# A three-stage token kernel: first tile's side channels spread by ScalarE, late weights loaded over two turns, the last tile's second layer moved to the first layer's buffers

## What is computed

```python
x_unf = x_pad[:, idx, :].reshape(B, S, K, H, group)   # seven shifted copies
x = np.einsum('hk,bskhg->bshg', softmax(weight), x_unf).reshape(B * S, 192)
h = x @ w_in                  # layer one: 192 -> 2048
x = (h * np.cos(h)) @ w_out   # 2048 -> 192
h = np.maximum(x @ w_in2, 0)  # layer two: 192 -> 2048
out = (h * h) @ w_out2        # 2048 -> 192
```

## Time and profile before

| | us |
|---|---|
| runs of the kernel, median of 3 | 2283.05 (2282.98 to 2283.62) |
| the profiled execution: its own time | 2284.51 |
| the profiled execution: its span, first to last instruction | 2282.7 |
| busy in the span: PE, DVE, ACT | 2237.8 (98%), 1779.4 (78%), 1695.5 (74%) |
| mean granted clock of TensorE | 0.994 of full speed |

### The profile page before, as it was taken

How to read it: one execution, slowest core, us unless ns; L and a number is a source line. 1 busy time by engine, 2 the same in 40 slices (tenths; PEclk the granted TensorE clock), 3 DMA queues, 4 the chain that set the end, 5 groups by cost and what they waited for, 6 DMA issues and landing times.

```text
span 2282.7 us, 47134 instructions
## 1 busy us (share of the span) xinstructions
PE 2237.8 (98%) x19456; PEld 1855.2 (81%) x19456; DVE 1779.4 (78%) x2003; ACT 1695.5 (74%) x1747; POOL 0.2 (0%) x4
## 2 busy tenths in 40 slices
PE   5899999999999999999999999999999999999998
PEld 4688888888888888888888888888888888888887
DVE  7877887777887778887778877778877778877762
ACT  5577777777777777777777777777777777777775
POOL 0000000000000000000000000000000000000000
PEclk9899999999999999999999999999999999999999
DMA  3100000000000000000000000000000000000000
GB/s 103 58 12 20 20 7 18 18 12 18 18 7 18 18 12 18 18 7 18 16 14 18 12 13 18 12 18 18 8 17 18 12 18 18 7 18 18 5 8 15
DMA packets 23696, 41.57 MB, mean 18 GB/s; under 512 B 3952, under 2 KB 12144, under 8 KB 23408
## 3 DMA queue, kind: packets, MB, share of 16 engines
q1 hardware_dynamic: 23520, 41.11, 6.5%
q10 hardware_dynamic: 144, 0.01, 0.0%
HBM read 20.13 MB, written 12.58 MB: 14 GB/s over the span
## 4 chain that ended last, share of the span: by engine, by line
PE 95%; DVE 2%; ACT 1%; DMA 1%; issue 0%; SPq 0%; DVEq 0%
PE h L316 10%; PE h L322 10%; PE h L320 10%; PE h L318 10%; PE y_B L353 5%; PE y_B L357 5%; PE y_B L359 5%; PE y_B L355 5%; PE y_B L361 5%; PE h L325 5%; PE y_A L353 5%; PE y_A L361 5%; PE y_A L359 5%; PE y_A L355 5%; PE y_A L357 5%
## 5 line engine op out<-in xcount | busy, mean ns | idle before, releaser
L586 DVE TENSOR_TENSOR g_lo<-g,g_hi 128x1024 fp32r<-128x1024 f32 x512 | 625.4, 1222 | 271.5 <-ACT g_hi L466 270.0
L466 ACT ACTIVATE g_hi<-g 128x1024 fp32r<-128x1024 f32 x512 | 537.3, 1050 | 41.6 <-DVE g L582 41.6
L458 ACT ACTIVATE w<-w,quarter 128x1024 f32<-128x1024 f32 x256 | 295.0, 1152 | 272.7 <-DVE w L576 272.7
L353 PE MATMUL y_A<-g_hi,dn_lo_A 64*128 64x512 f32 x1024 | 399.7, 390 | 9.8 <-DVE g_lo L586 9.8
L359 PE MATMUL y_A<-g_hi,dn_side_A 64*128 64x512 f32 x1024 | 398.5, 389 | 0.0
L355 PE MATMUL y_A<-g_hi,dn_hi_A 64*128 64x512 f32 x1024 | 398.1, 389 | 0.0
L361 PE MATMUL y_A<-g_lo,dn_side_A 64*128 64x512 f32 x1024 | 398.1, 389 | 0.0
L353 PE MATMUL y_B<-g_hi,dn_lo_B 64*128 64x512 f32 x1024 | 397.4, 388 | 0.4
L357 PE MATMUL y_A<-g_lo,dn_hi_A 64*128 64x512 f32 x1024 | 397.8, 388 | 0.0
L359 PE MATMUL y_B<-g_hi,dn_side_B 64*128 64x512 f32 x1024 | 396.9, 388 | 0.0
L355 PE MATMUL y_B<-g_hi,dn_hi_B 64*128 64x512 f32 x1024 | 396.4, 387 | 0.0
(11 more groups left out here) (85 smaller groups left out, 6082.7 us busy)
## 6 DMA issues: line engine op xcount, KB each, us to landing
xt<-x SPq DMA_DIRECT2D x32, 390.0 KB, 3.2
conv_both<-conv_side SPq DMA_DIRECT2D x128, 64.0 KB, 2.1
out<-late SPq DMA_DIRECT2D x32, 256.0 KB, 2.0
out<-late SPq DMA_DIRECT2D x32, 128.0 KB, 2.3
late<-w_out SPq DMA_DIRECT2D x2, 1536.0 KB, 10.2
late<-w_in SPq DMA_DIRECT2D x2, 512.0 KB, 4.2
late<-w_in SPq DMA_DIRECT2D x4, 256.0 KB, 5.6
w<-w_in SPq DMA_DIRECT2D x1, 768.0 KB, 6.7
```

What stands on the lines that cost most here:

```text
L353: mm = pe.matmul(y[kind][:, 0, :], dn_lo[kind][rows, c, :], hi, start=a, stop=False)
L466: act.activation(g_hi[:, s % RING, :, :], g[:, s % RING, :, :], ACT.Copy).then_inc(hi_made[kind], 1)
L586: dve.tensor_tensor(g_lo[:, r, :, :], g[:, r, :, :], g_hi[:, r, :, :].bitcast(F32), ALU.subtract).then_inc(lo_made[kind], 1)
```

## The change

Three edits. (1) In turn -1 the side channels of tile 0 are no longer unfolded by four DMAs but by six ScalarE copies of 64 partitions by 256 columns (`first_split`), which write `conv_both` and the rounded `x_side_A` directly; ScalarE's work on layer one's weights is put in another order around it, and the sine's table is loaded by a dummy instruction before it. VectorE's low parts of layer one's down weights move from turn -1 to behind the fractions of the first two A slots of turn 0. (2) The late weights come in the order first half of up, down, second half of up; the second half is loaded and split in turn 1 (ScalarE at slot 7, VectorE at slot 9); the first turn's taps start one slot earlier, and tile 1's input is split at slots 12 and 13 in place of 11 and 15. (3) Turn 31 gets a slot list of its own, in which the eighth A slot is slot 10 in place of 11; the last tile's layer-two input is made at slot 15 of turn 31, in `x_hi_A`, `x_lo_A`, `x_side_A` and a new `x_side_last`, and is summed in `y_A`; in turn 32 the B slots are slots 0 to 7.

```diff
-LAST_SLOTS = [("A", 0), ("B", 0), ("B", 1), ("B", 2), ("B", 3), ("B", 4), ("B", 5), ("B", 6),
-              ("B", 7), ("A", 1), ("A", 2), ("A", 3), ("A", 4), ("A", 5), ("A", 6), ("A", 7)]
+LAST_A_SLOTS = [("A", 0), ("A", 1), ("B", 0), ("A", 2), ("A", 3), ("B", 1), ("A", 4), ("A", 5),
+                ("B", 2), ("A", 6), ("A", 7), ("B", 3), ("B", 4), ("B", 5), ("B", 6), ("B", 7)]
+LAST_SLOTS = [("B", 0), ("B", 1), ("B", 2), ("B", 3), ("B", 4), ("B", 5), ("B", 6), ("B", 7),
+              ("A", 0), ("A", 1), ("A", 2), ("A", 3), ("A", 4), ("A", 5), ("A", 6), ("A", 7)]
-FIRST_TAP_SLOTS = (5, 6, 7, 8, 9, 10, 11)
+FIRST_TAP_SLOTS = (4, 5, 6, 7, 8, 9, 10)
+FIRST_SPLIT_SLOT, FIRST_LOW_SPLIT_SLOT = 12, 13
+LAST_Y1_SLOT = 15
-LATE_SLOTS, LATE_LOW_SLOTS = (6, 9, 13), (7, 10, 15)
+LATE_AT = {(0, 6): 1, (0, 13): 2, (1, 7): 3}
+LATE_LOW_AT = {(0, 7): 1, (0, 14): 2, (1, 9): 3}
...
+        def layer_in(turn, kind, back=0):
+            if turn.last(kind, back):
+                return xin_hi["A"], xin_lo["A"], xin_side["A"], xin_side_last
+            return xin_hi[kind], xin_lo[kind], xin_side[kind], xin_side_lo
...
@@ SP
-            spread_side(K)
             sp.wait_ge(tap_done, 2 * K)
             load_x(1)
-            for half in range(2):
-                sp.wait_ge(late_lo, 2 * half + 2)
...
+            sp.wait_ge(late_lo, 2)
+            load_layer2_up(0)
+            sp.wait_ge(late_lo, 4)
+            sp.wait_ge(even_made, 1)
+            sp.dma_start(stage_out, w2o.rearrange("p (c d) -> p c d", d=D)).then_inc(late_loaded, 16)
             spread_side(2 * 2 * K)
             load_x(2)
             sp.wait_ge(late_lo, 6)
-            sp.wait_ge(even_made, 2)
-            sp.dma_start(stage_out, w2o.rearrange("p (c d) -> p c d", d=D)).then_inc(late_loaded, 16)
+            load_layer2_up(1)
@@ PE
                 if turn.peeled and turn.i == 1 and p == 0 and kind == "B":
-                    pe.wait_ge(late_lo, 6)
+                    pe.wait_ge(late_lo, 4)
+                    pe.wait_ge(even_made, 1)
+                if turn.peeled and turn.i == 1 and p == NP // 2 and kind == "B":
+                    pe.wait_ge(late_lo, 8)
                     pe.wait_ge(even_made, 2)
...
                 if turn.peeled and turn.i - back == 1 and p == 0 and kind == "B":
-                    pe.wait_ge(late_lo, 8)
-                if kind == "B" and p == 0 and turn.runs("O"):
+                    pe.wait_ge(late_lo, 6)
+                if kind == "B" and p == 0 and turn.runs("O") and not turn.last(kind, back):
@@ ACT
+            act.wait_ge(zeroed, 1)
+            act.activation(unused[:, :], quarter[:, :], ACT.Sin)
...
+            def first_split():
+                act.wait_ge(tap_done, K)
+                parts = ((top, slice(0, HALF_TOK)), (low, slice(HALF_TOK, TOK)))
+                for half, part in parts:
+                    act.activation(conv_both[lo_rows["A"], part], conv_side[half, :], ACT.Copy)
+                    act.activation(xin_side["A"][hi_rows["A"], part], conv_side[half, :], ACT.Copy)
+                act.activation(xin_side["A"][lo_rows["A"], parts[0][1]], conv_side[top, :], ACT.Copy)
+                act.activation(xin_side["A"][lo_rows["A"], parts[1][1]], conv_side[low, :], ACT.Copy)\
+                   .then_inc(x1_hi, 1)
+                layer1_hi_side(1)
+                act.wait_ge(tap_done, 2 * K)
+                act.activation(xin_hi["A"][:, :], conv[:, :], ACT.Copy).then_inc(x1_hi, 1)
 
             def body(turn):
                 if turn.first:
-                    layer1_hi(0)
+                    layer1_hi_side(0)
+                    layer1_hi_main(0)
+                    first_split()
+                    layer1_hi_main(1)
+                    late_hi(0)
+                    return
                 for s, (kind, p) in enumerate(turn.slots()):
+                    if s == LAST_Y1_SLOT and turn.slots() is LAST_A_SLOTS:
+                        read_y1(turn, 0)
...
@@ DVE
                     layer1_up_lo(1)
-                    layer1_down_lo()
                     return
...
+                    if s == LAST_Y1_SLOT and turn.slots() is LAST_A_SLOTS:
+                        split_y1(turn, 0)
...
                     if kind == "A" and turn.runs("A"):
                         fraction(turn, s % RING, p)
-                    if turn.peeled and turn.i == 0 and s in LATE_LOW_SLOTS:
-                        late_lo_part(1 + LATE_LOW_SLOTS.index(s))
+                    if turn.peeled and turn.i == 0 and kind == "A" and p < 2:
+                        layer1_down_lo(p)
+                    if turn.peeled and (turn.i, s) in LATE_LOW_AT:
+                        late_lo_part(LATE_LOW_AT[turn.i, s])
```

More of the change, by code:

```diff
@@ L80, in slots, with last @@
             return FIRST_SLOTS
-        return LAST_SLOTS if self.peeled and self.i - back >= self.tiles else SLOTS
+        if self.peeled and self.i - back >= self.tiles - 1:
+            return LAST_SLOTS if self.i - back >= self.tiles else LAST_A_SLOTS
+        return SLOTS
+    def last(self, kind, back=0):
+        return kind == "B" and self.peeled and self.i - back == self.tiles
     def earlier(self, s, n):
@@ L244, in store_y, with load_layer2_up @@
                 sp.dma_start(out_tiles[t, P:D, :], yt_side).then_inc(y_stored, 16)
+            def load_layer2_up(half):
+                cols = slice(half * HALF, (half + 1) * HALF)
+                sp.dma_start(stage_main, w2i[0:P, cols]).then_inc(late_loaded, 16)
+                for rows in (top, low):
+                    sp.dma_start(stage_side[rows, :], w2i[P:D, cols]).then_inc(late_loaded, 16)
             load_x(0)
@@ L349, in down_step @@
                 c = p * PAIR + n
+                sums = layer_out(turn, kind, back)
                 hi, lo = g_hi[rows, r, n, :], g_lo[rows, r, n, :]
@@ L480, in read_y2 @@
                     act.wait_ge(y_stored, (turn.i - 2) * 32)
-                act.activation(yt_side, y["B"][low, 1, :], ACT.Copy).then_inc(y2_low, 1)
-                act.activation(yt, y["B"][:, 0, :], ACT.Copy).then_inc(y2_copied, 1)
+                sums = layer_out(turn, "B", 1)
+                act.activation(yt_side, sums[low, 1, :], ACT.Copy).then_inc(y2_low, 1)
+                act.activation(yt, sums[:, 0, :], ACT.Copy).then_inc(y2_copied, 1)
             def split_x1(turn):
@@ L501, in body @@
                         turned_cosine(turn, q, back)
-                    if s == Y1_SLOT and turn.runs("A", 1):
-                        read_y1(turn)
+                    if s == Y1_SLOT and turn.runs("A", 1) and turn.slots() is not LAST_SLOTS:
+                        read_y1(turn, 1)
                     if s == Y2_SLOT and turn.runs("O"):
@@ L649, in body @@
                     layer1_up_lo(1)
-                    layer1_down_lo()
                     return
+                split_at = FIRST_LOW_SPLIT_SLOT if turn.slots() is FIRST_SLOTS else LOW_SPLIT_SLOT
                 for s, (kind, p) in enumerate(turn.slots()):
-                    if s == Y1_SLOT and turn.runs("A", 1):
-                        split_y1(turn)
-                    if s == LOW_SPLIT_SLOT and turn.runs("C"):
+                    if s == Y1_SLOT and turn.runs("A", 1) and turn.slots() is not LAST_SLOTS:
+                        split_y1(turn, 1)
+                    if s == LAST_Y1_SLOT and turn.slots() is LAST_A_SLOTS:
+                        split_y1(turn, 0)
+                    if s == split_at and turn.runs("C"):
                         split_x1(turn)
@@ L667, in body @@
                             tap_main(turn, k, done + 2 * k - 1)
[L668 to L669 removed]
+                            if k == 0 and not (turn.peeled and turn.i == 0):
+                                dve.wait_ge(side_spread, turn.i * 64)
                             tap_side(turn, k, done + 2 * k)
```

104 lines of the change are left out of this document (52 added, 52 removed).

## The result

The changed kernel takes **2271.05 us** (2269.16 to 2271.70), 0.9944 of the time before (now 2283.34, of four runs), interval 0.9926 to 0.9961. So it is faster by about 12 us, where 16.35 were forecast, and stands 4.35 above the predicted 2266.7. The profiled execution took 2271.70, 12.8 less than the profiled execution before; its span, 2270.2, is 12.5 shorter. The busy times show little of it, since the work is the same: DVE's is unchanged, PE's 4.3 lower and ACT's 2.2 higher.

A forecast was written before the change was run, and what follows sets the result against it. PE, busy 98%, bounds the kernel, so only its stretches off pace (start, DVE-bound turn 0, end) can give time. Terms -12.5 + 2.25 - 6.1 = -16.35 from 2283.05 give 2266.7 us; range 2261.4 to 2276.0.

The forecast's parts named there:

- The start: Turn -1: six ACT copies replace four transfers, so PE's first matmul comes at 17.8 in place of 21.55.
- Turn 0: DVE-bound turn 0 ends earlier: slot 4 of turn 1 at 91.0 in place of 103.50; term -12.5 (-14 to -11).
- The chain up to the spread: Turn 0: DVE runs 3.3 us earlier, nothing waits for the spread, tile 0's last down slot at 73.1 for 84.57.
- Rival D: PE at 1.2 GHz, not DVE, bounds turns 0 and 1: +8.7, 2291.7 us; chance 0.04.
- Turn 1: Late weights delay the spread and B4's copy behind it, so PE waits in slot 14: +2.25 (0 to +4).
- rival B: PE's new waits in slot 14 and at turn 32 both lower its clock, 1.7 each: 2270.1 us; chance 0.14.
- The last tile: Turns 31 and 32: a wait of 1.5 replaces a half-filled slot and 3.67; term -6.1 (-7.6 to -4.4).
- Rival E: The last tile's edit gives nothing, ACT's queue holding `read_y1` back as before: 2272.8 us; chance 0.04.
- C: Turn 0 hands on only its head start, turn 1 coming 3.3 earlier and no more: 2275.9 us; chance 0.14.

The follow-up runs named there:

- the second profile: The changed kernel measured once more, nothing changed, profiled again with 3.4 us of low clock after 65 us and slot 4 of turn 1 at 90.11: median 2270.16 us.
- the extra matmuls: Changed kernel plus twelve PE matmuls with overwritten results ahead of each of slots 10 to 13 of turn 0, to keep the clock up: 2267.60 us.
- the last combined kernel: Changed kernel with tile 2's split at slot 13 of turn 1, `y_A` read ahead of B6's copy in the last tile, and turn 0's extra matmuls: 2261.83 us.

## Why the prediction was right in direction and 4.35 short

**Where the 4.35 went.** By the two profiled executions: slot 4 of turn 1 came 1.28 short of the forecast (11.22 for 12.5), turn 1 gave back 2.1 more than forecast (4.4 for 2.25), and the rest of the last tile gave 0.1 less. There ACT's copy of the output began 12.80 earlier, at 2265.64 for this row of the kernel before, and 12.80 - 6.83 = 5.97, for 6.1:

```profile
2278.44 0.59 ACT L481 ACTIVATE late<-y_B 64x512 f32<-64x512 f32 x1 [9.38 <-PE y_B L357]
```

The other 0.8 is no part of the kernel: the sum took off 1.46 to come from the profiled execution to the median, and the profiled execution after stood only 0.65 above its median.

**The start** held: the copies ended at 11.8, the side rows were released at 14.21 (14.1), PE started at 17.98 (17.8). DVE's idle time before the first fraction was 2.47 (3.2).

**Turn 0: a term of the sum that was mis-sized.** The chain up to the spread held: no wait of ACT for it, and with the clock kept the last down slot stands at 72.68 (73.1, though the addends shown make 72.9). The step that was mis-sized is "From there to A's first `h` of tile 1 it took 8.4 us (84.57 to 92.98), at the low clock for the most part. I take the same". The row of the kernel before that it rests on (columns as in the earlier trace rows):

```profile
83.10:90.00 6.90, 5.43 (x23) 4.37 (x24) 3.56 (x4) 3.02 (x3) 0.00 (x0) 0.51 0.43 180
```

There the low clock began 1.4 ahead of the last down slot, and it was taken over as a fixed length behind that slot. In the profiled execution after, it begins 3.9 ahead of it, under A's last but one, so PE itself delays the last (74.03), and slot 4 comes 3.4 later than with the clock kept. The prediction had a price for this in its own range, "14 earlier if the clock is full there": slot 4 then came at 88.89, 14.6 earlier. The 12.5 lay between the two cases that the changed kernel turned out to have. Against the profiles without edit 1, its head start was worth 0.46 at slot 4 in the execution with 10.2 us of low clock, 2.6 in the second profile and 2.4 with the clock kept.

**Rival D** is the mechanism of that, in a smaller place than it was given: PE at 1.2 GHz was the bound from 70 to 80, not in the whole of turns 0 and 1, and took 3.4 us where it lasted for 10, not 12.5.

**Turn 1: the other mis-sized term.** The wait, its place and its cause were right (2.50 for 2.25; between 1.90 and 3.15 in other executions). What failed is the step from wait to cost: half of rival B held. Behind the wait the clock was low for 3.4 us, which took some 1.6 (18 matmuls in 3.40 us; where the wait is gone, 34 fit into such a stretch). The two together make 4.1 of the 4.4 that the profiles show, and with the wait gone the way from slot 4 to B6's copy is again that of the kernel before, to 0.02. Where the wait came without a low clock behind it (edits 1 and 3 undone) that way was 3.3 and 3.2 longer than before.

**The last tile** was right in all its steps: the wait of 1.5, no low clock behind it, and 5.97 by the profiles, 5.7 by the run that undoes the edit. Rival E is out. So is C: slot 4 came 11 us earlier, far more than the head start.

**The rule of the Trainium skill** (TensorE: Matmul & The Clock Gate, HAM oscillation), that waits between bursts let the clock fall, was read as speaking for both halves of B. That section's own case has waits of some 3 to 5 us, longer than the two forecast here, so it said less for B than was taken from it. The traces show such a fall behind the wait in slot 14 in five of seven executions, and behind the wait of 1.50 at turn 32 in none of eight.

**What stays open.** Why the clock falls at the end of turn 0 in some executions and not in others of the same kernel was not settled. Of six profiles with edit 2 and without the extra matmuls, four had it low between DVE's product and the first fraction of tile 1; with the extra matmuls it stayed up there in all five.

## What to carry to other kernels

Where PE is starved, its own duration is not a constant: price the stretch at both levels of the clock, and see which engine is the bound at either, before a head start is carried through it. An engine's queue decides what a late transfer costs: a split that waits for one belongs behind the copies that free another engine's buffers. Extra matmuls into a buffer that is about to be overwritten are a cheap test of whether the clock is the limit, and here they were also worth keeping (2264.55 to 2261.83 in one group of runs). Two profiles are best compared from a point at which the engine that bounds them stands at the same time in both, not from the first matmul.

## What the runs showed that was not expected

The length of a wait alone does not tell whether the clock falls behind it. In slot 14, waits of 1.90 or 1.91 (three executions), 2.50 and 3.15 us were followed by 3.4 us at the low level, while waits of 2.87 (edit 3 undone) and 3.02 (edit 1 undone) were not. At turn 32, 1.50 us was never followed by it, and 3.68 was (edit 3 undone). And two profiled executions of the changed kernel had 10.2 and 3.4 us at the low level after 65 us, with nothing changed between them; with the extra matmuls no execution that was profiled had any from 65 us to slot 4 of turn 1, and the times of the last combined kernel lay within 1.1 us, for 4.9 without them. That is the widest contrast: the four other kernels with extra matmuls spread over 1.8 to 2.4 us, the others without over 1.4 to 4.4.
